# Experts and gated convolution in one program block, with a down product for every convolution unit

## The reference

```python
# 1: a delta-rule attention over 768 tokens, 2 batches, 8 heads of 48
# 2: each token goes to one of 8 experts e
h = np.maximum(x[b, s] @ w1[e], 0.0)          # 384 -> 1024
out[b, s] = p[e] * (h @ w2[e])                # 1024 -> 384
# 3: gated convolution over the sequence
h = np.maximum(x @ w_in, 0.0)                 # 384 -> 1024
for k in range(3):
    conv_out += conv_w[k][None, None, :] * hp[:, k:k + S, :]
gate = 1.0 / (1.0 + np.exp(-conv_out))
return (h * gate @ w_out)                     # 1024 -> 384
```

## Time and profile before

| | |
|---|---|
| median of 3 runs | 629.13 us (620.86 to 629.34) |
| profiled execution | 630.51 us, span 629.0 us |
| mean granted TensorE clock | 0.783 of full |
| busy, share of span | PE 81%, DVE 59%, ACT 45%, POOL 21% |
| last expert matmul ends | 480.16 us |
| convolution: first gather to end | 487.46 to 629.0 us |

### The profile page before, as it was taken

One profiled execution on the slowest core, in us unless ns is written; L12 is line 12 of the kernel. 1 busy time (PEld: TensorE's weight loads), 2 busy tenths in 40 slices (PEclk: granted clock), 3 DMA queues, 4 the chain that ended last, 5 costly groups with the idle time before them and its releaser, 6 DMA issues. The chain is left out here.

```text
span 629.0 us, 16845 instructions
## 1 busy us (share of the span) xinstructions
PE 507.8 (81%) x6996; PEld 463.8 (74%) x6996; DVE 373.8 (59%) x524; ACT 285.0 (45%) x463; POOL 132.0 (21%) x148
## 2 busy tenths in 40 slices
PE   6728889698979996203999999999994689769998
PEld 5627767587868885102898998999993479659997
DVE  4593446324451102742799999999972548996460
ACT  4204223121213222312899999999971225543241
POOL 4322231030500000382011111011000704552130
PEclk9766566656557556555999999999998579989999
DMA  7734510101000002356277655564000400000002
GB/s 132 133 67 113 182 28 3 28 4 29 5 3 3 4 3 70 143 201 209 84 248 250 225 198 177 190 211 150 25 26 25 143 9 1 0 2 24 28 27 75
DMA packets 60833, 54.65 MB, mean 87 GB/s; under 512 B 41155, under 2 KB 54339, under 8 KB 60774
## 3 DMA queue, kind: packets, MB, share of 16 engines
q1 hardware_dynamic: 55750, 41.37, 22.2%
q0 software_dynamic: 3968, 12.19, 5.7%
q10 hardware_dynamic: 1056, 0.20, 0.2%
HBM read 76.16 MB, written 12.19 MB: 140 GB/s over the span
## 5 line engine op out<-in xcount | busy, mean ns | idle before, releaser
L1380 DVE TENSOR_TENSOR w2l<-raw,w2h 128x768 fp32r<-128x768 f32 x76 | 67.8, 955 | 6.6 <-ACT w2h L1323 6.6
L1380 DVE TENSOR_TENSOR w1l<-raw,w1h 128x1024 fp32r<-128x1024 f32 x54 | 63.0, 1220 | 2.7 <-ACT w1h L1323 0.6
L1323 ACT CAST w2h<-raw 128x768 fp32r<-128x768 f32 x76 | 58.2, 851 | 0.7 <-DMA raw<-in_moe_w_dram 0.7
L1439 PE MATMUL ps<-w2h,hh 128*128 128x384 f32 x152 | 52.3, 344 | 1.8 <-DVE hl L1385 1.8
L1323 ACT CAST w1h<-raw 128x1024 fp32r<-128x1024 f32 x54 | 53.6, 1066 | 0.4 <-DMA raw<-in_moe_w_dram 0.2
L1441 PE MATMUL ps<-w2h,hl 128*128 128x384 f32 x152 | 50.8, 334 | 0.0
L1440 PE MATMUL ps<-w2l,hh 128*128 128x384 f32 x152 | 50.8, 334 | 0.0
L1539 POOL TENSOR_TENSOR gate<-h,gate 128x768 f32<-128x768 f32 x16 | 34.4, 2152 | 75.2 <-ACT gate L1558 75.2
L1422 PE MATMUL ps<-w1h,xh 128*128 128x512 f32 x114 | 47.4, 416 | 1.6 <-DVE xl L1372 1.6
L1613 DVE TENSOR_SCALAR cv<-h,cw 128x768 f32<-128x768 f32 x16 | 28.7, 1792 | 28.8 <-ACT gate L1558 22.1
L1424 PE MATMUL ps<-w1h,xl 128*128 128x512 f32 x114 | 45.7, 401 | 0.0
(11 more groups left out here) (213 smaller groups left out, 1181.8 us busy)
## 6 DMA issues: line engine op xcount, KB each, us to landing
raw<-in_moe_w_dram SPq DMA_DIRECT2D x57, 512.0 KB
raw<-in_moe_w_dram SPq DMA_DIRECT2D x76, 384.0 KB
x_sorted<-zeros SPq DMA_DIRECT2D x1, 3648.0 KB, 12.8
x_all<-x_sorted POOLq DMA_DIRECT2D x19, 192.0 KB, 2.7
y_sorted<-x_all POOLq DMA_DIRECT2D x19, 192.0 KB, 2.2
q_nat<-in_q_dram SPq DMA_DIRECT2D x24, 96.0 KB, 3.0
v_nat<-in_v_dram SPq DMA_DIRECT2D x24, 96.0 KB, 2.9
out_dram<-res SPq DMA_DIRECT2D x12, 192.0 KB, 1.8
```

The costliest lines, as they stand in the source:

```text
L1323: act.copy(hi(par), raw).then_inc(s_wh, 1)
L1380: dve.tensor_tensor(lo(par), raw, hi(par).bitcast(F32), ALU.subtract).then_inc(s_wl, 1)
L1439: pe.matmul(psY[par], hh[:, i, c], w2h[:, par, f], start=(f == 0), stop=False)
```

## The change

**One block.** `experts` and `gated_conv` write into the same program block. The barrier between them is gone, and so is POOL's wait at the end of `experts`: it now stands in front of the gathers, which alone need it. The other engines wait for what they read: DVE and PE for `s_y` (all results taken from PSUM), ACT for the gathers. The convolution's weights are loaded at the start of `experts`, into rows of `x_all` that `experts` doesn't use, and gather 8 waits until they have been turned (`s_cc`).

**The start of the convolution.** `scale` moves from DVE to ACT. PE runs extra matmuls that nothing reads (`warm`): 16 before and 16 after the turning of the convolution's weights, and 2 behind most `turn`s. Units 0 and 1 have their first halves done early, while the second half of the tokens is still being gathered. On ACT the two relus of these halves stand among the scalings of the pieces, here pieces 5 to 10 (`h<-ps` are the relus):

The diff, cut to its core:

```diff
@@ experts, gpsimd
-            pool.wait_ge(s_yd[0], 16 * ((NT + 1) // 2))
-            pool.wait_ge(s_yd[1], 16 * (NT // 2))
@@ gated_conv
+    LAG = 2
+    SLOTS = 4
+        psH = [ps[:, i, 0:CW] for i in range(NCH)]
+        psO = [ps[:, NCH + i, 0:DM] for i in range(NPB)]
@@ gpsimd
+            pool.wait_ge(s_yd[0], 16 * ((NT + 1) // 2))
+            pool.wait_ge(s_yd[1], 16 * (NT // 2))
             for n in range(NSTEP):
+                if n == CW_ROW:
+                    pool.wait_ge(s_cc, 1)
                 pool.indirect_dma_start(...)
-            for i in range(NU):
-                pool.wait_ge(s_sg, i + 1)
-                pool.tensor_tensor(gate[:, i % 3], h[:, i % 4, 1:S + 1], gate[:, i % 3], ALU.mult).then_inc(s_gg, 1)
@@ scalar
+            for n in range(NSTEP):
+                scale(n)
+                if n:
+                    high_x(n - 1)
+                if n == NS:
+                    relu(0, 0)
+                if n == NS + 2:
+                    relu(1, 0)
+            high_x(NSTEP - 1)
+            relu(0, 1)
+            relu(1, 1)
+            for i in range(2, NU + 2):
+                for j in range(NCH):
+                    if i < NU:
+                        relu(i, j)
+                    if j == 0:
+                        sigmoid(i - 2)
+                high(i - 2)
+                if i == CF + LAG:
+                    for n in range(TPB):
+                        store(n)
@@ vector
             for i in range(NU + 2):
                 if i < NU:
+                    conv_first(i)
+                if 1 <= i <= NU:
+                    gated(i - 1)
+                if i < NU:
+                    conv_next(i, 1)
+                if 1 <= i <= NU:
+                    low(i - 1)
                 if i < NU:
                     conv_next(i, 2)
@@ tensor
+            def warm(count):
+                for i in range(count):
+                    pe.matmul(ps[:, NCH + NM, 0:P], ident[:], ident[:], start=True, stop=True)
+            def down(i):
+                b, f = units[i]
+                slot = i % SLOTS
+                pe.wait_ge(s_gl, i + 1)
+                for t in range(TPB):
+                    ts = slice(t * P, (t + 1) * P)
+                    if b and f == 0:
+                        pe.wait_ge(s_res, t + 1)
+                    pe.matmul(psO[t], gh[:, slot, ts], woh[:, f], start=(f == 0), stop=False)
+                    pe.matmul(psO[t], gh[:, slot, ts], wol[:, f], start=False, stop=False)
+                    pe.matmul(psO[t], gl[:, slot, ts], woh[:, f], start=False, stop=(f == CF - 1)).then_inc(s_op, 1)
+            for i in range(2, NU + 1):
+                if i < NU:
+                    for j in range(NCH):
+                        up(i, j)
+                down(i - LAG)
+            down(NU - 1)
```

More of the change, by code:

```diff
@@ L1252, in w2_split @@
             return j * NC + 2 * CD + (c - CD)
-        block = ctx.enter_context(nc.Block())
         @block.sync
@@ L1541, in _, with scale, high_x @@
         @block.scalar
         def _(act):
-            for n in range(NSTEP):
+            def scale(n):
+                act.wait_ge(s_gt[n], 16)
+                act.activation(x_all[:, n, :], x_all[:, n, :], ACT.Copy, scale=prob[:, n:n + 1]).then_inc(s_sc, 1)
+            def high_x(n):
                 act.wait_ge(s_mt, n + 1)
[L1545 to L1552, removed]
+                act.copy(mh[:, n].rearrange("p c b t -> p (c b t)"), psM[n % NM]).then_inc(s_mh, 1)
@@ L1554, in sigmoid, with relu @@
+            def relu(i, j):
+                act.wait_ge(s_hp, chunk(i, j) + 1)
+                if i >= NH and j == 0:
+                    act.wait_ge(s_gg, i - NH + 1)
+                act.activation(h[:, i % NH, 1 + j * CW:1 + (j + 1) * CW], psH[chunk(i, j) % NCH],
+                               ACT.Relu).then_inc(s_hs, 1)
             def sigmoid(i):
                 act.wait_ge(s_cn[KW - 1], i + 1)
-                if i >= 3:
-                    act.wait_ge(s_gl, i - 2)
-                act.activation(gate[:, i % 3], cv[:, i % 2], ACT.Sigmoid).then_inc(s_sg, 1)
+                if i >= 2:
+                    act.wait_ge(s_gg, i - 1)
+                act.activation(gate[:, i % 2], cv[:, i % 2], ACT.Sigmoid).then_inc(s_sg, 1)
@@ L1562, in high, with down_done @@
                 if i >= SLOTS:
-                    act.wait_ge(s_op, TPB)
-                act.copy(gh[:, i % SLOTS], gate[:, i % 3]).then_inc(s_gh, 1)
+                    act.wait_ge(s_op, down_done(i - SLOTS))
+                act.copy(gh[:, i % SLOTS], hg[:, i % 2]).then_inc(s_gh, 1)
             def store(n):
[L1567 to L1581, removed]
+                act.wait_ge(s_op, down_done((n // TPB + 1) * CF - 1, n % TPB))
+                if n >= NRES:
+                    act.wait_ge(s_out[n % NRES], 16 * (n // NRES))
+                act.copy(res[:, n % NRES], psO[n % TPB]).then_inc(s_res, 1)
+            def down_done(i, t=TPB - 1):
+                return i * TPB + t + 1
+            for n in range(NSTEP):
[19 more added lines that the diff above has]
+                        store(n)
             for n in range(TPB, B * TPB):
@@ L1601, in _ @@
             for n in range(NSTEP):
[L1602 to L1605, removed]
+                low_x(n)
             dve.wait_ge(s_pad, 2)
             dve.wait_ge(s_cc, 1)
[L1609 to L1625, removed]
@@ L1667, in up @@
                 m.then_inc(s_hp, 1)
[L1669 to L1680, removed]
-                if f1 == CF:
-                    m.then_inc(s_op, 1)
@@ L1687, in _ @@
+            pe.wait_ge(s_y, NT)
+            warm(16)
+            pe.wait_ge(s_cw, 16)
+            for f in range(CF):
+                t = pe.transpose(psW[:, f * KW:(f + 1) * KW], cw_r[:, f * P:(f + 1) * P], ident[0:KW, 0:KW])
+            t.then_inc(s_ct, 1)
+            warm(16)
+            for n in range(NS):
                 turn(n)
-            pe.wait_ge(s_ml, early)
+                warm(2)
+            pe.wait_ge(s_cc, 1)
+            pe.wait_ge(s_ml, NS)
             up(0, 0)
-            for n in range(early + 2, NSTEP):
+            turn(NS)
```

137 lines of the change are left out of this document (71 added, 66 removed).

## The result

The changed kernel takes 680.61 us, the median of 4 runs (678.6 to 682.22), beside 629.24 for the kernel before on the same chip. The ratio is 1.0861 [1.0778, 1.0944]: slower by 8.6%. That ratio times the 629.13 us that the forecast started from makes 683 us; forecast were 672, with 649 to 682. The direction and the mechanism in the units were right; the start and the size weren't.

A forecast was written before the change was run, and what follows sets the result against it. It took batch 0 to be paced by DVE and the rest by PE. Full clock with PE's stops gave 651 us on the median's scale; clock falls added 21, making 672 us, range 649 to 682.

The forecast's parts named there:

- The boundary: Between last store and first gather: the gather starts at 483.5 instead of 487.46, gain 4.0 us (0 to 4.3).
- The rival that it keeps its price: At the block boundary: at worst the first gather starts as late as now, gain 0; no chance of its own.
- The units at full clock: In each middle unit: a 4.14 us chain from relu(i, 0) stops PE for 2.55 us; a unit takes 9.18 us.
- The clock: In the units: 13 of 14 stops make PE's clock fall, 1.65 us lost each, 21.5 us in all.
- the clock holds: Rival for the units: stops leave the clock at full speed; 651 us (649 to 655), chance 0.20.
- every fall lasts as long as the two seen: In the units: low clock for some 6.1 us per fall would lose 2.7 us each; no chance given.
- The stop doesn't form: Rival for the units: low(i - 2) is ready when up(i, 1) ends, PE runs through; about 609 us, chance 0.05.
- up(0, 1) starts at 505.0: End of the gathering: summed landings, scalings and turns put up(0, 1) at 505.0 instead of 508.36, gain 3.4 us.
- The range: For the whole kernel's time: 649 to 682 us, meant to hold 8 in 10; over 682 had 0.06.

The follow-up runs named there:

- the order alone: Changed kernel with only ACT's order edited: sigmoid(i - 1) behind both relus of unit i, high(i - 2) in front; 617.63 us, ratio 0.9821 to the kernel before.
- second repeat: The changed kernel run again without any edit, beside the kernel before; 672.68 us, ratio 1.0691.
- the two later repeats: The changed kernel run twice more without any edit, each beside the kernel before; 672.68 us and 668.96 us.

## Why the prediction missed

- **The boundary**: 2.43 us from store to gather in all four traces, forecast 2.5. The rival that it keeps its price is refuted.
- **The units at full clock**: stop 2.58 for 2.55, chain 4.13 for 4.14, unit 9.18 for 9.18, 146.5 us for 145.6. That the stop comes from the sigmoid's place behind relu(i, 0) is shown by the order alone: changed, it is gone from the middle units.
- **The clock**: 12 falls for 13, 1.5 us each ((164.7 - 146.5) / 12) for 1.65: 18 us for 21.5. In the first trace the clock came back after 3.4 us at the lower level in 11 of the 12, and after 6.8 in one. The rivals "the clock holds" and "every fall lasts as long as the two seen" (6.0 and 6.1) are refuted. The Trainium skill, page "TensorE: Matmul & The Clock Gate", section "HAM oscillation — how this bites in real kernels", lays a fall to longer gaps than these 2.58 us; here the measurement decides against it.
- **"The stop doesn't form" (609)** is what the changed order makes: 617.6. It named the condition (the sigmoid doesn't depend on relu(i, 0)). From up(0, 1) to the end it has 98.8 us of matmuls and 5 for the end, 103.8, where 111.54 were measured: it left out the first stop (2.42), the fall of the clock behind it, and the wait of down(8) for a result to be copied (1.77).
- **The step that failed** is "up(0, 1) starts at 505.0", 21.5 us behind the first gather. It was a sum of landings and durations with no allowance either way. In three traces it holds to 0.6 us, though two of its terms were off: scaling on ACT takes 0.62, not 0.49, and a `warm` matmul is two records, 0.24 us and not 0.117, so that 32 take 7.7 us and not 3.7. They weren't hidden: in the second repeat piece 0 was scaled at 487.16 and turned from 488.83 on. In the trace of the result it was 32.07 and up(0, 1) started at 513.02: ACT waited 3.6, 3.3 and 3.3 us for signals of PE, 10.2 us in all, and every piece behind them came later. The forecast had no term for a signal that comes late.
- **The range** ended at 682 because only mechanisms of the units were in it. The same kernel's executions lie between 662 and 682, and its last store, ahead of the convolution, is issued between 478.5 and 485.1. The forecast took the one value 480.97. The spread of those stages alone (3.3 us to either side) would have carried the upper end to 685. That the repeats come out at 672.7 and 669.0, beside a forecast of 672, is in part luck: the units of their traces took up to 5.4 us less than forecast and the last store came up to 2.3 us later (4.1 in the first).

What stays open is why the signals were late. The traffic of DMA in the 18 us behind the first gather isn't different (131 to 133 GB/s in both halves, as in the second repeat), PE had done its work, and it shows in one trace only of the ten that have the scaling on ACT. Each late `mh` started 1.4 to 1.6 us after the `warm` pair behind the next turn had ended, but the other traces with these pairs have no late signal, so that neither clears nor blames them. How much of the first comparison's 680.6, against 669 to 673 of the two later repeats, is due to it can't be told: runs without a trace don't show it.

## What to carry to other kernels

An engine that works in order ties every instruction to what the one in front waits for: before moving work to another engine or tile, write out for each in-order engine which instruction of a later unit stands in front of an earlier unit's chain. Where a chain has several hops and the consumer must not stop, put its first link one unit earlier, not its last one faster. A stop is paid twice, as time and as clock: filling it with matmuls gave back the second part (20 us here), a better order both (55). And where a forecast takes one trace's time for the stages that it doesn't touch, their spread from run to run belongs in the range.

## What the runs showed of the hardware

- Stops of 2.58 us (the first of 4.00) brought the clock down 12 times in 14. It stayed at the lower level for 3.4 us in 11 cases and 6.8 in one, where the earlier trace rows have 6.0 and 6.1, one behind short stops and one behind a stop of 4.79. A stop of 1.77 to 1.84 us, the one before down(8), was followed by a fall in two traces (product on POOL; no `warm`) and by none in two others (changed order; scaling on DVE).
- A 128x128 matmul of f32 by `ident` is two records of 0.12 us: 18 records for 9 matmuls in 2.17 us.
- A `tensor_tensor` on POOL takes 2.03 to 2.67 us beside DVE's `conv_next`, and 1.54 in the last unit, at 608.48, where DVE stood still; `conv_next` itself stays at 1.02. In the kernel before it was `conv_first` that grew, to 2.18; with the new order it is over (0.62) before POOL starts.
- ACT's `mh` started 2.8, 6.3 and 6.6 us after the turns that it waited for, three times in one traced execution and in no other.
